# A routed expert layer after an attention scan: first gates in the common table, w1 of the second expert in places of its own, and a new order of GpSimd's work before the first tile

## The reference, cut to what matters

```python
x = attention(r, k, v, w, u)                 # 3072 tokens x 384
logits = x @ w_gate                          # 3072 x 8
e_idx = argmax(logits); probs = softmax(logits)
gate_w = probs[n, e_idx]; eom = sigmoid(x @ w_output_gate)
for e in range(8):                           # w1: 384 x 1024, w2: 1024 x 384
    mask = e_idx == e
    out[mask] = gate_w[mask] * eom[mask, e] * (relu(x[mask] @ w1[e]) @ w2[e])
y = relu(out @ w_in) ** 2 @ w_out            # 384 -> 2048 -> 384
```

## Time and profile before

| | |
|---|---|
| three runs | 918.13, 920.03, 922.46 us; median 920.03 |
| the profiled execution's own time | 915.25 us |
| its span | 913.5 us |
| TensorE (PE) busy | 877.8 us |
| attention / routing to the first tile / experts / dense layer | 0 to 222 / 222 to 257.6 / 257.6 to 505.9 / 505.9 to 913.5 us |

### The profile page before, as it was taken

The page is one execution under the profiler, slowest core; times in us unless marked ns, Lnnn a source line. Parts: engine busy times, 40 slices in busy tenths (PEclk is TensorE's granted clock), DMA queues, the critical chain, the costliest instruction groups (busy, mean ns, idle before and its releaser), DMA issues.

```text
span 913.5 us, 26366 instructions
## 1 busy us (share of the span) xinstructions
PE 877.8 (96%) x10791; PEld 802.4 (88%) x10792; DVE 487.1 (53%) x868; ACT 390.3 (43%) x725; POOL 155.8 (17%) x111
## 2 busy tenths in 40 slices
PE   5889999999989999999999999999999999999995
PEld 4789999997779999999999789899899899899895
DVE  7679999999754244334333670550640641631620
ACT  4467777777442243224323650540530620621510
POOL 1000000000283545254425101000001001001000
PEclk9899999999789999999999999999999999999998
DMA  7356666672174764565468410010010010000000
GB/s 292 118 179 245 241 242 241 244 258 77 31 237 132 168 164 81 182 165 162 77 190 186 83 36 27 9 34 26 9 43 17 9 43 26 0 9 26 1 17 18
DMA packets 45182, 99.21 MB, mean 109 GB/s; under 512 B 11904, under 2 KB 32032, under 8 KB 41184
## 3 DMA queue, kind: packets, MB, share of 16 engines
q1 hardware_dynamic: 40240, 86.02, 30.2%
q0 software_dynamic: 3936, 11.60, 4.5%
q10 hardware_dynamic: 976, 1.18, 0.4%
HBM read 83.84 MB, written 14.96 MB: 108 GB/s over the span
## 4 chain that ended last, share of the span: by engine, by line
PE 90%; DVE 3%; issue 2%; POOL 1%; ACT 0%; POOLq 0%; DVEq 0%; ACTq 0%
PE y_banks L1357 22%; PE h_banks L1347 22%; PE h_banks L1318 13%; PE y_banks L1331 12%; PE yt L320 5%; PE yt L342 4%; PE ms L354 3%; PE sc L262 3%; PE sc L257 2%; PE ms L282 2%; PE xt_ps L1299 1%; PE ms L294 1%; POOL W L1006 1%; PE sc L269 1%; PE sc L260 1%
## 5 line engine op out<-in xcount | busy, mean ns | idle before, releaser
L1357 PE MATMUL y_banks<-W,g 128*128 128x384 f32 x1152 | 200.8, 334 | 0.0
L1357 PEld LDWEIGHTS y_banks<-W,g 128*128 128x128 f32 x1152 | 200.0, 188 | 0.5
L1347 PE MATMUL h_banks<-yT,W 128*128 128x512 f32 x864 | 198.9, 392 | 0.8 <-POOL yT L1258 0.8
L1347 PEld LDWEIGHTS h_banks<-yT,W 128*128 128x128 f32 x864 | 162.1, 188 | 36.2 <-issue 1.2
L1422 ACT ACTIVATE relu<-h_banks 128x512 f32<-128x512 f32 x96 | 57.5, 599 | 235.0 <-PE h_banks L1347 235.0
L1318 PE MATMUL h_banks<-xT,W 128*128 128x448 f32 x576 | 119.7, 369 | 2.8 <-POOL W L1006 2.8
L1331 PE MATMUL y_banks<-h,W 128*128 128x448 f32 x576 | 120.9, 368 | 0.0
L1318 PEld LDWEIGHTS h_banks<-xT,W 128*128 128x128 f32 x576 | 109.4, 190 | 11.7 <-issue 3.0
L1331 PEld LDWEIGHTS y_banks<-h,W 128*128 128x128 f32 x576 | 107.0, 188 | 8.7
L1499 DVE TENSOR_TENSOR relu<-relu 128x512 f32<-128x512 f32 x96 | 66.5, 692 | 68.3 <-ACT g L1426 67.9
L1517 DVE COPY stage<-y_banks 128x384 f32<-128x384 f32 x24 | 13.4, 558 | 164.9 <-PE y_banks L1357 164.9
(11 more groups left out here) (171 smaller groups left out, 1016.9 us busy)
## 6 DMA issues: line engine op xcount, KB each, us to landing
stage<-in_w SPq DMA_DIRECT2D x16, 1536.0 KB, 7.6
V<-in_vs SPq DMA_DIRECT2D x16, 1296.0 KB, 7.9
RK<-in_rkw SPq DMA_DIRECT2D x15, 1160.0 KB, 5.2
y_columns<-y_sb SPq DMA_DIRECT2D x8, 672.0 KB, 3.6
x_rows<-xs SPq DMA_DIRECT2D x32, 144.0 KB, 6.9
yb<-y_columns SPq DMA_DIRECT2D x5, 768.0 KB, 4.4
stage<-in_w_in SPq DMA_DIRECT2D x2, 1536.0 KB, 9.7
stage<-in_w_out SPq DMA_DIRECT2D x2, 1536.0 KB, 10.8
```

The source lines that it names most:

```text
L1347: ins = pe.matmul(h_ps[f % BANKS][:], w_in_of[wp][:, f // NF1, k, f % NF1 * P:(f % NF1 + 1) * P], yT[yp][:, k, :], start=(k == 0 and i == ...
L1357: ins = pe.matmul(y_ps[s % 2][:, 0:X], g[gp][:, f, s * P:(s + 1) * P], w_out_of[wp][:, f, :], start=(f == 0 and i == 0), stop=(f == NF2 - ...
```

## The change

Five edits. (1) The first tile's gates no longer have a table of their own: their 8 columns stand ahead of the other 156 in `others`, and the one table of 164 columns (L1048) gives `scale_now` too; eight `stay_warm` products stand where two, the table of gates and four stood. DVE spreads the gates quarter by quarter behind each quarter of L927, and makes the last quarter of the numbers in ACT's place. (2) w1 of expert 2 is loaded into three tensors `raw` of its own, as soon as x has been stored; ACT and DVE make its parts from there, and ACT no longer waits for the buffer. (3) Since it doesn't pass through `stage`, SyncE loads w1 of expert 3 into `stage` where w1 of expert 2 was loaded; the later loads of w1 follow one expert earlier in the same waits. (4) POOL gathers the second tile's rows first and makes the low part of the first w2 after that. (5) TensorE waits for w2 at the first product of the y stage and no more at the start of the expert. SyncE, ACT and DVE have the first two experts written out ahead of their loops.

```diff
@@ routing @@
+    GATES = 2 * SUB
+    others = sb("others", [P, TILES, GATES + 3 * REST], F32R)
...
@@ DVE in routing @@
-        spread_over(first_spread[:], the_first, slice(0, TILES)).then_inc(first_spread_ready, 1)
+        spread_over(0, the_first, slice(0, TILES))
         for q in range(4):
             ...  in_part of the rest, ALU.is_equal).then_inc(part_ready, 1)
+            dve.wait_ge(part_ready, q + 1)
+            spread_over(GATES, the_rest, some).then_inc(spread_ready, 1)
+        some, shape = slice(3 * QUARTER, TILES), [P, QUARTER, REST]
+        vec.tensor_tensor(others[:, some, GATES + 2 * REST:], in_part[:, some, the_rest], over(token[:, some], shape), ALU.mult).then_inc(numbers_ready[1], 1)
...
-        dve.wait_ge(first_scaled, 1)
-        link(vec.tensor_copy(scale_now[:], first_scale_ps[:, 0:SUB]))
-        vec.tensor_tensor(scale_now[:], scale_now[:], first_scale_ps[:, SUB:2 * SUB], ALU.add).then_inc(scale_ready, 1)
-        for q in range(4):
-            some = slice(q * QUARTER, (q + 1) * QUARTER)
-            dve.wait_ge(part_ready, q + 1)
-            spread_over(others[:, some, 1:], the_rest, some).then_inc(spread_ready, 1)
+        dve.wait_ge(tabled, 1)
+        link(vec.tensor_copy(scale_now[:], tab_ps[:, 0:SUB]))
+        vec.tensor_tensor(scale_now[:], scale_now[:], tab_ps[:, SUB:GATES], ALU.add).then_inc(scale_ready, 1)
@@ SyncE in routing @@
+        sp.wait_ge(step, 1)
+        sp.wait_ge(x_stored, 4 * 16 * 2 * B + STORED_AHEAD)
+        for k in range(KX):
+            sp.dma_start(raw[k][:], w1[1, k * P:(k + 1) * P, :]).then_inc(raw_loaded, 16)
-        for half, m in enumerate((w1, w2)):
+        for half, m in enumerate((w1[2], w2[1])):
             sp.wait_ge(w_ready[half], PIECES[half])
-            load_half(sp, stage, half, m[1], stage_loaded)
+            load_half(sp, stage, half, m, stage_loaded)
@@ GpSimd in routing @@
-        pool.wait_ge(w_ready[0], PIECES[0])
-        pool.wait_ge(hi_ready, HI_PIECES)
-        nc.gpsimd.tensor_tensor(W0[:, 1, HALF_W:], stage[:, HALF_W:], W0[:, 0, HALF_W:].bitcast(F32), ALU.subtract).then_inc(w_ready[1], PIECES[1])
@@ TensorE in routing @@
-        stay_warm(2)
-        pe.wait_ge(first_spread_ready, 1)
-        for t in range(TILES):
-            ins = pe.matmul(first_scale_ps[:, 0:2 * SUB], in_row[:, t, :], first_spread[:, t].rearrange("p i c -> p (i c)"), ...)
-        ins.then_inc(first_scaled, 1)
-        stay_warm(4)
+        stay_warm(8)
         for t in range(TILES):
             if t % QUARTER == 0:
-                pe.wait_ge(numbers_ready, t // QUARTER + 1)
-                pe.wait_ge(spread_ready, t // QUARTER + 1)
-            ins = pe.matmul(tab_ps[:, 0:3 * REST], in_row[:, t, :], others[:, t].rearrange("p i c -> p (i c)"), ...)
+                q = t // QUARTER
+                pe.wait_ge(spread_ready, q + 1)
+                pe.wait_ge(numbers_ready[q // 3], q % 3 + 1)
+            ins = pe.matmul(tab_ps[:, 0:GATES + 3 * REST], in_row[:, t, :], others[:, t], ...)
@@ ACT in routing @@
-        for t in range(TILES):
+        for t in range(3 * QUARTER):
@@ tiles: experts written out @@
-        with eng.Fori(0, E // 2 - (1 if peeled else 0)) as e2:
+        for e in range(first):
+            expert(e % 2, e)
+        with eng.Fori(first // 2, E // 2 - (1 if peeled else 0)) as e2:
@@ SyncE, prepare @@
             for half in range(2):
-                sp.wait_ge(w_ready[half], (e + 2) * PIECES[half])
-                sp.sem_inc(carrier, 1)
-                load_half(sp, stage, half, halves[half], stage_loaded)
+                if half or not isinstance(e, int) or e:
+                    sp.wait_ge(w_ready[half], (e + 2) * PIECES[half])
+                    sp.sem_inc(carrier, 1)
+                    load_half(sp, stage, half, halves[half], stage_loaded)
@@ GpSimd, after the second tile's gather @@
+        pool.wait_ge(x_scaled, SUB)
+        nc.gpsimd.tensor_tensor(W[0][:, 1, HALF_W:], stage[:, HALF_W:], W[0][:, 0, HALF_W:].bitcast(F32), ALU.subtract).then_inc(w_ready[1], PIECES[1])
@@ TensorE, weights and tile @@
-            pe.wait_ge(w_ready[1], (e + 1) * PIECES[1])
-            pe.sem_inc(carrier, 1)
...
+                    if c + f == 0:
+                        pe.wait_ge(w_ready[1], (e + 1) * PIECES[1])
+                        pe.sem_inc(carrier, 1)
@@ ACT, prepare @@
-            act.wait_ge(stage_loaded[0], (e + 2) * 16)
-            act.wait_ge(y_full, t0 * KX + Y_AHEAD)
+            if isinstance(e, int) and e == 0:
+                act.wait_ge(raw_loaded, KX * 16)
+            else:
+                act.wait_ge(stage_loaded[0], (e + 1) * 16)
+                act.wait_ge(y_full, t0 * KX + Y_AHEAD)
-                nc.scalar.copy(W[1 - b][:, 0, cols], stage[:, cols]).then_inc(w_hi, 1)
+                nc.scalar.copy(W[1 - b][:, 0, cols], staged_w1(e, i)).then_inc(w_hi, 1)
```

More of the change, by code:

```diff
@@ L810, in routing @@
     row_ready, first_ready, first_tabled = sem("row_ready"), sem("first_ready"), sem("first_tabled")
-    first_spread_ready, first_scaled = sem("first_spread_ready"), sem("first_scaled")
-    part_ready, numbers_ready, spread_ready, tabled = sem("part_ready"), sem("numbers_ready"), sem("spread_ready"), sem("tabled")
+    part_ready, numbers_ready = sem("part_ready"), [sem(f"numbers_ready{i}") for i in range(2)]
+    spread_ready, tabled = sem("spread_ready"), sem("tabled")
     ids_ready, hi_ready = sem("ids_ready"), sem("hi_ready")
@@ L898, in rows_of, with spread_over @@
             vec.tensor_tensor(in_row[:, some], over(row[:, some], shape), each(rows[:], shape), ALU.is_equal).then_inc(row_ready, 1)
-        def spread_over(out, columns, some):
-            shape = [P, some.stop - some.start, 2, columns.stop - columns.start]
+        def spread_over(at, columns, some):
+            width = columns.stop - columns.start
+            shape = [P, some.stop - some.start, 2, width]
+            out = others[:, some, at:at + 2 * width].rearrange("p t (i c) -> p t i c", i=2)
             return vec.tensor_tensor(out, in_part[:, some, columns].rearrange("p t (o c) -> p t o c", o=1).to_broadcast(shape),
@@ L1143, in w2_of, with staged_w1, tiles @@
         return W[b][:, part, HALF_W:].rearrange("p (k f) -> p k f", k=NF1)
+    def staged_w1(e, i):
+        return raw[i][:] if isinstance(e, int) and e == 0 else stage[:, i * PIECE:(i + 1) * PIECE]
     w_in_of = [W[0][:, i, :].rearrange("p (c k f) -> p c k f", c=2, k=KX) for i in range(2)]
     w_out_of = [W[1][:, i, :].rearrange("p (k f) -> p k f", k=NF2) for i in range(2)]
-    def tiles(eng, tile, before=None, peeled=False):
+    def tiles(eng, tile, before=None, peeled=False, first=0):
         def expert(b, e):
@@ L1184, in prepare @@
         def prepare(b, e, t0):
-            if isinstance(e, int):
+            if isinstance(e, int) and e >= E - 2:
                 halves = ((w_in[:, 0:F1], w_in[:, F1:]), (w_out[0:F1, :], w_out[F1:, :]))[b]
@@ L1207, in tile @@
             sp.dma_start(id_dram[bass.ds(at + whole * P, PART_ROWS[whole]), :], scatter_now[0:PART_ROWS[whole], whole:]).then_inc(ids_stored, 16)
-        tiles(sp, tile, before=prepare, peeled=True)
+        tiles(sp, tile, before=prepare, peeled=True, first=2)
         sp.wait_ge(ids_stored, S_AHEAD + tiles_of_all(sp) * ID_STORES)
@@ L1245, in prepare, with tile @@
             nc.gpsimd.tensor_tensor(new[:, 1], staged, new[:, 0].bitcast(F32), ALU.subtract).then_inc(w_ready[1], PIECES[1])
-        def tile(b, at, g):
+        def tile(b, e, at, g):
             pool.wait_ge(xt_full, (g + AHEAD) * HALVES)
@@ L1401, in _ @@
         act.wait_ge(meta_ready, 1)
-        tiles(act, tile, before=prepare)
+        tiles(act, tile, before=prepare, first=2)
         act.wait_ge(needed_ready, 1)
@@ L1463, in prepare, with tile @@
                 dve.wait_ge(w_hi, e * PIECES[0] + i + 1)
-                nc.vector.tensor_tensor(W[1 - b][:, 1, cols], stage[:, cols], W[1 - b][:, 0, cols].bitcast(F32),
+                nc.vector.tensor_tensor(W[1 - b][:, 1, cols], staged_w1(e, i), W[1 - b][:, 0, cols].bitcast(F32),
                                         ALU.subtract).then_inc(w_ready[0], 1)
-        def tile(b, at, g):
+        def tile(b, e, at, g):
             for f in range(NF1):
@@ L1487, in _ @@
         dve.wait_ge(meta_ready, 1)
-        tiles(dve, tile, before=prepare)
+        tiles(dve, tile, before=prepare, first=2)
         def y_lo(m):
```

44 lines of the change are left out of this document (20 added, 24 removed).

## The result

The changed kernel takes 912.50 us (median of 5 runs, 907.42 to 914.22) against 920.03 (5 runs, 918.13 to 922.46). The ratio is 0.990, 95% interval 0.986 to 0.994. Taken again in a later job it was 909.77 (4 runs) against 918.98: 0.991, 0.988 to 0.994. So the change gives about 1%: 7.5 us by the first medians, 9.2 by the second; 5.6 were forecast. Executions of either kernel lie several us apart. The lowest of the 100 of the kernel before on record is 913.71, the lowest of the 9 of the changed kernel 907.42, 6.3 us less.

What follows compares the result with a forecast made beforehand. Rows and w2, ending almost together, were taken to bound the first h stage; moving both starts the first y stage at 269.1 instead of 274.7, so 920.03 - 5.6 = 914.4 us, range 911.0 to 918.5.

Steps and rivals of the forecast that it cites:

- The sum: Whole kernel: first y stage starts at 269.1 instead of 274.7, 5.6 us less, median 914.4 us.
- Part 1: Gate tables ahead of the first tile: one table at half clock, ending at 245.6 instead of 250.59 us.
- Part 4: Later loads, third tile's gather and stores: w2 of expert 2 done at 284.1, 15 us free; all fits.
- Part 3: Own places for w1 of expert 2: loads cost nothing and gain nothing on PE.
- What bounds the kernel: Ahead of the first h stage: rows at 256.27 and w2 at 257.11 end together; moving w2 alone gives under 1 us.
- rival A: Clock at the tables: full clock back about 241, y stage at 267, gain 7.3 us, 912.7; chance 0.12.
- Part 2: w2's low part behind the second gather: h stage from 252.0, subtraction done 268.0, PE asks 269.1, 1 us slack.
- Rival B: First tile: slow gather issues, table waits and idle time give half back; gain 2.5 to 4.5 us; chance 0.23.
- rival C: Second tile: DVE's L1464 held by POOL's subtraction through the shared port; 920.4, a little slower; chance 0.06.

Runs made afterwards that it cites:

- via_stage: Changed kernel with w1 of expert 2 loaded through the common buffer again, ACT waiting for it; 920.08 us, ratio 1.003.
- late_wait: Kernel before with only TensorE's wait for w2 moved to the first product of the y stage; 916.09 us, ratio 0.998.
- w2_first: Changed kernel with GpSimd's old order, the first w2's low part ahead of the second tile's rows; 914.75 us, 0.996.
- no_table: Changed kernel with the separate table of first gates and the old order of DVE and ACT back; 917.11 us, 0.999.
- stage_ordered: Changed kernel with w1 of expert 2 through the common buffer and POOL's first w2 subtraction waiting for that w1's low part; 912.05 us, 0.993.
- warm2: Changed kernel with two idle products instead of eight ahead of the common table; 912.25 us, 0.993.
- before_again: Kernel before, unchanged, a second profile; 918.85 us, ratio 1.000.
- after_again: Changed kernel, unchanged, a second profile; 909.77 us.

## Why the prediction was right or wrong, point by point

5.6 us were forecast, 7.5 and 9.2 were measured. Three steps failed. The sum was mis-sized in Part 1: its table ran at half clock, with rows and h stage 29.9 us behind the first operation, where the first profile had the clock back and 28.1, so that the first y stage gained 7.2 us. Part 4 let the third gather land in time, where PE lost 1.4 us to it. And Part 3 gave the new places of w1 no worth on PE, where via_stage lost 10.7 us without them; this one did not enter the sum. The first two point opposite ways: at equal pace the first pair of profiles differs by 5.9 us, so that the forecast lies near it partly by luck. What the medians gain beyond that is not traced.

- **What bounds the kernel: two of four.** Rows and w2 were both named. The third bound, DVE behind POOL's port inside the h stage, was not, though its row was read: L960 was costed at the 0.5 us that it lost there. Nor was the fourth, the load of w1 of expert 2. late_wait shows that an h stage 4.1 us earlier gains nothing at the y stage while it stands.
- **Part 1.** DVE's chain was right: the table of the changed kernel could start its last quarter 21.6 us behind the first operation, forecast 243.5 - 222.1 = 21.4. "PE runs quarters at half clock" failed for the first profile: there a quarter took 0.87 us, the table ended at 22.6 instead of 245.6 - 222.1 = 23.5, and with faster transposes the h stage began at 28.1 where 29.9 was forecast. That was rival A, and the other profile of the same code went the forecast's way (29.4). Both exist, 1.3 us apart. At the first y stage 5.6 us were forecast; 5.9 and 7.2 came.
- **Part 2.** Right in its times: the subtraction was done 43.9 us behind the first operation, forecast 268.0 - 222.1 = 45.9, and 1.8 of the 2.0 between are the earlier rows; slack 1.2 us, forecast 1. Wrong in what the new order is for: it was weighed by w2's time and the 0.5 us of L960 only. w2_first puts it at 6.0 us, by the port and the half clock behind it.
- **Part 3, the step most wrong in its cause.** "Gain nothing on PE either, since L1389 and L1464 were hidden." Hidden they were in the old place; with the h stage 7 us earlier the load that they wait for is not. via_stage loses 10.7 us without its own places, 6.6 of them only for want of an order between POOL and DVE. The step took a cover from the trace of before and didn't ask whether it still lies over the moved work.
- **Part 4.** "All of it fits" failed for the third gather. Issue was forecast to end at about 290 and landing by the usual 3 us; it landed in 13.5, under 1.5 MB of w2, 0.7 MB of stores and the next w1. ACT stood 5.2 to 6.2 us in three profiles of this order, and second h stage to third took 1.4 to 1.9 us longer than before. Under no_table ACT stood 3.4 us and PE lost nothing.
- **Rival B** was right in kind for a part (something given back behind the first tile), and **rival C** was not met: L1478 of the second tile began 1.65 us after its h stage, w2 landed in 7.2 us. Its mechanism, however, was there, in the first tile. The Trainium skill, SBUF — State Buffer, "Who interferes with whom", says that the pair of ports is held for the whole instruction and that the other engine stands: the runs agree, with 5.22 us for 0.19, 6.56 for 0.16, both ending within 0.05 us of POOL's instruction, and 10.32 for 3.5. So the rule that I put behind the second tile's rival was the bound of the first. That `gather_now` would stand until the end of the subtraction for expert 2 was not met in the changed kernel: it took 1.88 us, ended with POOL's cast at 279.30, and was through before the subtraction began at 279.36. In stage_ordered it stood as said.
- **The sum.** 5.6 us stood against 7.5 (0.6% against 1.0% by the ratio). The traces give less. The first pair differs by 4.1 us at the first dense product, and by 5.9 with the slow pace's 1.8 us taken off; before against warm2, both without the slow pace and both at half clock in the table, by 4.3. The second pair can't be set side by side so, since before_again ran slow from the second tile and after_again in the first and second only. So 1.6 to 3.2 of the 7.5 us are not traced to the change, and more of the 9.2. Executions differ by up to 2.9 us by the pace (283.8 and 286.7 for the kernel before) and 4.8 by the start of the routing. Whether the change alters how often either occurs can't be said from 14 profiles, and stays open.
- **The working.** Two slips changed nothing. The upper end of the range, rival B's 917.5 with 1.5 us of scatter, is 919.0 and not 918.5; and 1.77 us behind a tile that ends at 284.5 is 286.3 and not 286.1.

That the parts need each other can be read off the first y stage of single profiles: 1.0 us for the table alone, 0.0 for the wait alone, 7.2 for all, and 3.3, 6.0 and 10.7 lost when table, order or places are taken out. The order alone, the places alone and the change without TensorE's late wait were not run.

## What to carry to other kernels

When several edits move one stage earlier, "hidden" must be asked again for each wait of that stage at its new place: a load, a port, a queue that was long over is now in the way. A small DVE instruction that takes twenty times its length behind a GpSimd one may be a bound (3.71 us in late_wait and 5.22 in w2_first held PE up, 6.56 in stage_ordered did not): look at what DVE does next and who waits for that. Order the two engines so that GpSimd's long SBUF instructions meet none of DVE's two-input ones or SBUF copies. A transfer that is moved past others has to be priced by what it then shares the DMA engines with, ahead and behind.

## What the runs showed that was not expected

Matmul pairs of 448 columns came at two paces at the same granted clock of 1.00: 72 products in 14.60 or in 14.88 us, 48 in 9.93 or 10.11, while the first 24 of a y stage took 4.87 in both. The change from one to the other comes in the middle of a tile and mostly lasts to the end of the experts; it was seen behind the first tile in 7 of 14 profiles, of the old code and the new. What brings it on was not found. And the clock came back before the end of the table in some executions and not in others of the same code: after and after_again, and 6 of 9 profiles that have eight idle products ahead of the one table.
